# Expert stage of a fused attention and mixture-of-experts kernel: the loop over two rounds of four experts becomes eight bodies, with slot counts read ahead and with loads that wait for their own buffer

## What is computed

```python
def _moe2_ref(x, w_skip, w_gate, w1, w2):
    do_compute = x @ w_skip > 0
    out = x.copy()
    xc = x[do_compute]
    logits = xc @ w_gate
    e_idx = np.argmax(logits, axis=1)
    ...
    for e in range(E):                       # E = 8
        mask = e_idx == e
        h = np.maximum(xc[mask] @ w1[e], 0.0)      # w1[e]: 384 x 1024
        y[mask] = gate_w[mask, None] * (h @ w2[e]) # w2[e]: 1024 x 384
    out[do_compute] = xc + y
```

## Time and profile before

| | |
|---|---|
| median of 3 runs | 970.22 us (968.25 to 970.82) |
| the profiled execution's own time | 968.83 us |
| its span | 966.9 us |
| TensorE busy (matmuls) | 751.7 us, 78% of the span |
| VectorE busy | 699.2 us, 72% |
| ScalarE busy | 367.4 us, 38% |
| mean granted clock of TensorE | 0.922 of full speed |
| each w1 or w2 load of the expert stage | 1536 KB |
| first load of the expert stage issued | 766.68 us into the span |
| first and last start of an expert slot | 805.06 and 951.08 us |

### The profile page before, as it was taken

The page is one execution under the profiler, slowest core; times in us unless marked ns, Lnnn a source line. Parts: engine busy times, 40 slices in busy tenths (PEclk is TensorE's granted clock), DMA queues, the critical chain, the costliest instruction groups (busy, mean ns, idle before and its releaser), DMA issues. The chain is left out here.

```text
span 966.9 us, 16131 instructions
## 1 busy us (share of the span) xinstructions
PE 751.7 (78%) x5478; PEld 723.3 (75%) x5479; DVE 699.2 (72%) x1231; ACT 367.4 (38%) x805; POOL 51.8 (5%) x48
## 2 busy tenths in 40 slices
PE   1343456987897989889798889979999547998786
PEld 1333456987886989788688788879999447998786
DVE  6967988988999799898899989875333373434333
ACT  5452234435434534433453353334433222322221
POOL 1000000000000000000000000000000012233122
PEclk9999567999999899999999999999999857999799
DMA  6542343243342424424242352233210393324520
GB/s 188 178 152 79 93 118 90 64 130 113 80 109 62 139 65 115 126 66 133 70 118 73 100 151 63 70 113 97 57 56 1 133 357 110 126 73 163 205 82 17
DMA packets 82433, 104.74 MB, mean 108 GB/s; under 512 B 15990, under 2 KB 68384, under 8 KB 82336
## 3 DMA queue, kind: packets, MB, share of 16 engines
q1 hardware_dynamic: 80544, 99.69, 35.2%
q0 software_dynamic: 1792, 3.76, 1.2%
HBM read 61.04 MB, written 12.19 MB: 76 GB/s over the span
## 5 line engine op out<-in xcount | busy, mean ns | idle before, releaser
L524 PE MATMUL out_ps<-w_out_hi,g_parts 128*128 128x394 f32 x768 | 225.3, 350 | 26.3 <-DVE g_parts L933 26.3
L514 PE MATMUL mlp_ps<-xT,w_in_hi 128*128 128x384 f32 x768 | 207.1, 351 | 20.3 <-DMA xT<-y_parts 8.6
L524 PEld LDWEIGHTS out_ps<-w_out_hi,g_parts 128*128 128x128 f32 x768 | 145.9, 193 | 30.3 <-DVE g_parts L933 30.2
L514 PEld LDWEIGHTS mlp_ps<-xT,w_in_hi 128*128 128x128 f32 x768 | 140.5, 194 | 27.5 <-issue 13.5
L928 DVE SCALAR_TENSOR_TENSOR g<-mlp_ps,slope_side,bent 128x384 f32<-128x384 f32 x128 | 78.6, 615 | 83.4 <-ACT bent L666 75.3
L524 PE MATMUL out_ps<-w_out_lo,g_parts 128*128 128x394 f32 x384 | 133.8, 348 | 0.0
L514 PE MATMUL mlp_ps<-xT,w_in_lo 128*128 128x384 f32 x384 | 131.2, 342 | 0.0
L666 ACT ACTIVATE bent<-mlp_ps,bend_size 128x384 f32<-128x384 f32 x128 | 73.7, 576 | 149.5 <-PE mlp_ps L514 149.0
L1303 PE MATMUL mlp_ps<-xT_e,w_sb 128*128 128x128 f32 x624 | 79.5, 290 | 19.3 <-issue 14.1
L1303 PEld LDWEIGHTS mlp_ps<-xT_e,w_sb 128*128 128x128 f32 x624 | 77.4, 205 | 22.1 <-issue 16.9
L672 ACT ACTIVATE g_parts<-g 128x384 fp32r<-128x384 f32 x128 | 66.2, 517 | 35.4 <-DVE g L928 35.4
(11 more groups left out here) (150 smaller groups left out, 1082.8 us busy)
## 6 DMA issues: line engine op xcount, KB each, us to landing
kq<-qk_dec SPq DMA_DIRECT2D x96, 144.0 KB, 3.0
w_sb<-in_w SPq DMA_DIRECT2D x8, 1536.0 KB, 7.7
w_raw<-in_w SPq DMA_DIRECT2D x8, 1536.0 KB, 12.0
gates<-in_a SPq DMA_DIRECT2D x24, 384.0 KB, 4.3
qk_raw<-in_qk SPq DMA_DIRECT2D x24, 384.0 KB, 4.2
xT<-y_parts SPq DMA_DIRECT2D x48, 144.0 KB, 2.8
v_nat<-in_v SPq DMA_DIRECT2D x24, 192.0 KB, 4.0
out<-x SPq DMA_DIRECT2D x8, 576.0 KB, 3.2
```

Of the source, the lines that this page charges most:

```text
L514: last = pe.matmul(ps[:, 0:HT], w_in_v[s][:, kk, f * P:(f + 1) * P], xT[n.p][:, kk, m, :], start=(kk == 0 and j == 0), stop=(kk == KT - 1 ...
L524: last = pe.matmul(out_ps[i][:, 0:DL], g_parts[:, f % 4, s, i * P:(i + 1) * P], w_out_v[m][:, f, :], start=(f == 0 and j == 0), stop=(f == ...
```

## The change

The loop over i is gone: `for e in range(EXPERTS)` in Python writes out eight bodies on each engine. All eight slot counts are read into registers ahead of the first expert. TensorE no longer raises `expert_done`; VectorE raises `expert_left` at the end of each expert, when it has made that expert's last `y`. On SyncE the w2 load of a second-round expert is issued ahead of its w1 load and waits for `w2_lo` alone; the w1 load waits for `expert_left` of the expert whose buffer it overwrites.

```diff
-        def expert(x, i, p):
-            if isinstance(i, int):
-                return x[BODY * i + p:BODY * i + p + 1]
-            return x[bass.ds(i * BODY + p, 1)]
-        def slots_of(eng, i, p):
-            return eng.value_load(slots_i[0:1, bass.ds(i * BODY + p, 1)], min_val=0, max_val=NJ)
+        def expert(x, e):
+            return x[e:e + 1]
+        def slots_of_all(eng):
+            return [eng.value_load(slots_i[0:1, e:e + 1], min_val=0, max_val=NJ) for e in range(EXPERTS)]
...
-            def load(i, p):
-                if i > 0:
-                    sp.wait_ge(expert_done, i * BODY + p - (BODY - 3))
-                    sp.wait_ge(w1_loaded[p], 16 * i)
-                sp.dma_start(w1_v[p][:, :, :], expert(w1, i, p).rearrange("e (k p) f -> p (e k) f", p=P)).then_inc(w1_loaded[p], 16)
-                if i > 0:
-                    sp.wait_ge(w2_lo, i * BODY + p - (BODY - 1))
+            def load_w1(e):
+                p = e % BODY
+                if e >= BODY:
+                    sp.wait_ge(expert_left, e - BODY + 1)
+                    sp.wait_ge(w1_loaded[p], 16 * (e // BODY))
+                sp.dma_start(w1_v[p][:, :, :], expert(w1, e).rearrange("e (k p) f -> p (e k) f", p=P)).then_inc(w1_loaded[p], 16)
+            def load_w2(e):
+                p = e % BODY
+                if e >= BODY:
+                    sp.wait_ge(w2_lo, e - BODY + 1)
                 sp.dma_start(w2_raw[p][:, :, :],
-                             expert(w2, i, p).rearrange("e (f p) d -> p (e f) d", p=P)).then_inc(w2_loaded[p], 16)
-            for p in range(BODY - 1):
-                load(0, p)
+                             expert(w2, e).rearrange("e (f p) d -> p (e f) d", p=P)).then_inc(w2_loaded[p], 16)
+            for e in range(BODY - 1):
+                load_w1(e)
+                load_w2(e)
             sp.wait_ge(table_full, 1)
-            load(0, BODY - 1)
-            for i in range(1, EXPERTS // BODY):
-                for p in range(BODY):
-                    load(i, p)
+            load_w1(BODY - 1)
+            load_w2(BODY - 1)
+            for e in range(BODY, EXPERTS):
+                load_w2(e)
+                load_w1(e)
+            for p in range(BODY):
+                sp.wait_ge(w1_loaded[p], 16 * (EXPERTS // BODY))
...
-            until = pe.alloc_register("pe_slot_of_expert_before")
-            pe.reg_mov(until, 1)
             pe.wait_ge(slots_known, 1)
+            slots_here = slots_of_all(pe)
             pe.wait_ge(x_gathered, 16)
             turn_x()
...
-                pe.wait_ge(b_done, pe.snap(until, min_val=1, max_val=NSLOT - 1))
-                pe.sem_inc(expert_done, 1)
-                pe.reg_mov(until, count)
-            with pe.Fori(0, EXPERTS // BODY) as i:
-                for p in range(BODY):
-                    expert_slots(i, p)
+            for e in range(EXPERTS):
+                expert_slots(e)
...
-            def split(i, p):
-                if not (isinstance(i, int) and i == 0):
-                    act.wait_ge(expert_done, i * BODY + (p - 1))
-                act.wait_ge(w2_loaded[p], val(i * 16 + 16))
+            def split(e):
+                p = e % BODY
+                if e >= BODY:
+                    act.wait_ge(expert_left, e - BODY + 1)
+                act.wait_ge(w2_loaded[p], e // BODY * 16 + 16)
                 act.activation(w2_v[p][0][:, :, :], w2_raw[p][:, :, :], ACT.Copy).then_inc(w2_hi, 1)
             count = act.alloc_register("act_slot")
             act.reg_mov(count, 1)
-            split(0, 0)
-            split(0, 1)
+            split(0)
+            split(1)
+            act.wait_ge(slots_known, 1)
+            slots_here = slots_of_all(act)
             place_x(1)
-            act.wait_ge(slots_known, 1)
-            def expert_slots(i, p):
-                n = slots_of(act, i, p)
+            def expert_slots(e):
+                n = slots_here[e]
                 def split_next():
-                    if p < BODY - 2:
-                        split(i, p + 2)
-                    else:
-                        with act.If(i < EXPERTS // BODY - 1):
-                            split(i + 1, p + 2 - BODY)
-                        act.nop()
+                    if e + 2 < EXPERTS:
+                        split(e + 2)
...
+                dve.sem_inc(expert_left, 1)
```

More of the change, by code:

```diff
@@ L1195, in phase2 @@
         w2_lo = sem("w2_lo")
-        expert_done = sem("expert_done")
+        expert_left = sem("expert_left")
         x_gathered = sem("x_gathered")
@@ L1284, in _ @@
             pe.reg_mov(count, 1)
-            until = pe.alloc_register("pe_slot_of_expert_before")
-            pe.reg_mov(until, 1)
             pe.wait_ge(slots_known, 1)
+            slots_here = slots_of_all(pe)
             pe.wait_ge(x_gathered, 16)
             turn_x()
-            def expert_slots(i, p):
-                n = slots_of(pe, i, p)
+            def expert_slots(e):
+                n, p, i = slots_here[e], e % BODY, e // BODY
                 def slot(is_first=False):
@@ L1297, in slot @@
                     if is_first:
-                        pe.wait_ge(w1_loaded[p], val(i * 16 + 16))
+                        pe.wait_ge(w1_loaded[p], i * 16 + 16)
                     for g in range(NP):
@@ L1310, in slot @@
                     if is_first:
-                        pe.wait_ge(w2_hi, val(i * BODY + (p + 1)))
-                        pe.wait_ge(w2_lo, val(i * BODY + (p + 1)))
+                        pe.wait_ge(w2_hi, e + 1)
+                        pe.wait_ge(w2_lo, e + 1)
                     for f in range(NFE):
@@ L1385, in expert_slots @@
                 act.nop()
-                with act.If(n < 1):
-                    split_next()
+                if e + 2 < EXPERTS:
+                    with act.If(n < 1):
+                        split_next()
+                        act.nop()
                     act.nop()
-                act.nop()
                 over_slots(act, n, slot)
-            with act.Fori(0, EXPERTS // BODY) as i:
-                for p in range(BODY):
-                    expert_slots(i, p)
+            for e in range(EXPERTS):
+                expert_slots(e)
         @block.vector
@@ L1510, in keep_x, with split @@
                 dve.tensor_copy(x_kept_rows[:, bass.ds(s % 2, 1), :].rearrange("p a d -> p (a d)"), x_in[:, :]).then_inc(x_kept, 1)
-            def split(i, p):
-                dve.wait_ge(w2_hi, val(i * BODY + (p + 1)))
+            def split(e):
+                p = e % BODY
+                dve.wait_ge(w2_hi, e + 1)
                 dve.tensor_tensor(w2_v[p][1][:, :, :], w2_raw[p][:, :, :], w2_v[p][0][:, :, :].bitcast(F32), ALU.subtract).then_inc(w2_lo, 1)
@@ L1521, in _ @@
             dve.tensor_copy(scatter_at[:, :], tab[:, NSLOT - 1, 0:1]).then_inc(first_at, 1)
-            split(0, 0)
+            split(0)
+            dve.wait_ge(slots_known, 1)
+            slots_here = slots_of_all(dve)
             keep_x(1)
@@ L1525, in _, with expert_slots @@
             dve.reg_mov(count, 1)
-            dve.wait_ge(slots_known, 1)
             dve.wait_ge(step, val(last_step))
-            def expert_slots(i, p):
-                n = slots_of(dve, i, p)
+            def expert_slots(e):
+                n = slots_here[e]
                 def split_next():
[L1533 to L1538, removed]
+                    if e + 1 < EXPERTS:
+                        split(e + 1)
                 def slot(is_first=False):
@@ L1563, in expert_slots @@
                 dve.nop()
-                with dve.If(n < 1):
-                    split_next()
+                if e + 1 < EXPERTS:
+                    with dve.If(n < 1):
+                        split_next()
+                        dve.nop()
                     dve.nop()
-                dve.nop()
                 over_slots(dve, n, slot)
-            with dve.Fori(0, EXPERTS // BODY) as i:
-                for p in range(BODY):
-                    expert_slots(i, p)
+                dve.sem_inc(expert_left, 1)
+            for e in range(EXPERTS):
+                expert_slots(e)
         @block.gpsimd
         def _(pool):
-            pool.sem_inc(expert_done, 1)
             pool.sem_inc(b_done, 1)
```

## The result

The changed kernel takes 956.74 us (median of 4 runs, 954.14 to 957.86) against 969.41 for the kernel before in the same comparison: a ratio of 0.9877 with a 95% interval from 0.9848 to 0.9906. It is faster by 12.7 us (9.1 to 14.7 by that interval), where 19.7 were forecast (970.22 to 950.5); the time lies 0.7 us above the forecast range.

A forecast was written before the change was run, and what follows sets the result against it. TensorE bounds the 13 slots (busy 137.67 of 156.40 us); 1.98 + 1.0 + 6.10 + 2.73 + 5.15 + 3 x 1.02 − 0.7 = 19.3 us off 968.83 gives 949.5, the median 1.4 higher: 950.9, stated as 950.5, range 946.5 to 956.

The forecast's parts named there:

- Loads of w2: Second-round w2 loads come 15 us or more early; gaps inside slots 5, 8, 11 go: 1.98, about 1.0, slot 11 separately.
- The loop's branch: Behind slot 8, TensorE's 6.58 us passage shrinks to 0.48: 6.10 us, plus 2.73 for slot 9's first layer at full clock.
- The end of each expert: Wait, increment and count go from TensorE's passages: 1.02 us each where the sequencer is late, counted for slots 3, 9, 12.
- The far jumps stay: TensorE's jumps over unused bodies at experts' ends remain, each passage kept as it was, 3.46 us over three bodies.
- Slot 11: Without the wait and slow matmuls it takes 11.08 instead of 16.23 us: 5.15 gained, including its own 1.02.
- The counts ahead: Eight slot-count reads before the first expert, 5.4 us on each engine, are hidden by other waits: nothing taken.
- The first, a fetch that stays: Rival: the loop branch's 4.90 us moves to expert 4's entry, losing 4.9 + 2.7 us, time 958; chance 0.08.
- the second: Rival: expert 4's w2 delays the first gather, awaited by slot 1, some 4 us once or twice: 954 to 958; chance 0.08.
- the clock was low only behind idle times: Rival: TensorE's clock is lowered for being busy without gaps, 5.5 us more per slot, 972 to some 1004; chance 0.03.
- no split waits any more: Rival: ScalarE's splits waited for expert_done, not the load, so gaps stay: some 5 us less gain, 955.5; chance 0.04.
- signs of being wrong: Idle over 2 us ahead of slot 9 or 10, first gather landing after 804, or transposes awaiting gathers in several slots.
- The rule of the Trainium skill: Code comes in 256-instruction blocks; jumps outside a two-block window wait: expert 5's turns short, 0 short, 3 long, 1 us more.

The follow-up runs named there:

- loop_new_loads: The kernel before, with its loop and counts in place, given the new loads only (w2 first, w1 told by VectorE): 965.42 us, ratio 0.9999.
- counts_in_place: Changed kernel with each slot count read at the start of its expert on the three engines, as before: 958.90 us, one run.
- pad40: Changed kernel with 40 increments of an unused semaphore on TensorE ahead of expert 0, moving expert code by 39 places: 954.25 us, ratio 0.9874.
- pad140: Changed kernel with 140 semaphore increments on TensorE ahead of expert 0: 967.0 us, one run.
- calm: Changed kernel, SyncE alone altered: expert 5's w2 issued ahead of expert 4's w1, which waits until expert 1 is left: 955.20 us, ratio 0.9886.
- old_loads: Changed kernel's eight bodies and counts ahead, but second-round loads in the order and with the waits of before: 960.57 us, ratio 0.9938.
- paced_pad40: pad40 with second-round loads one by one, each held until the next slot's gather has landed: 949.47 us, ratio 0.9817.
- late_pair: calm with expert 6's w1 and expert 7's w2 held until seven slots are done: 957.18 us, one run.
- paced2: Changed kernel with loads held one by one for gathers, in another order than paced_pad40's, no increments added: 953.13 us, ratio 0.9840.
- paced2_pad40: paced2's loads with the 40 increments on TensorE: 948.19 us, ratio 0.9803.

## Why the prediction was wrong

By its own steps, against the changed kernel's slots:

- **Loads of w2: right in mechanism and in place.** All were issued within some 3 us of the forecast, the gaps in slots 5, 8 and 11 are gone. In loop_new_loads, though, the loads alone gain nothing that the time shows (ratio 0.9999), because of what follows.
- **The loop's branch: right.** Slots 8 and 9 take 10.68 and 10.90 us where 10.8 and 10.83 were worked out; 10.9 us gained.
- **The end of each expert: right but for the jumps.** 1.02 us a passage, of which 0.67 is the count's; counts_in_place puts back 0.66 to 0.89 for that part once its jumps' own differences are taken off.
- **"The far jumps stay": this is the step that failed.** They stayed in number, but their price was taken from an execution in which no load was in flight at them, and the same change moved loads onto one. Slots 3 and 4 were worked out at 11.08 and 10.7 us (with the 0.7 for the gather, a wait that no run here shows in slot 4) and took 13.82 and 12.55: 4.6 us lost. In the five kernels with loads in flight there (changed, pad40, pad140, loop_new_loads, counts_in_place) the jump took 6.16 to 6.42 us; in the five with none (before, calm, old_loads, paced_pad40, late_pair) 3.42 to 3.74; in the two paced2 kernels, where the end of one w1 load reaches into it (12.2% and 9.3% of the DMA engines' time), 3.88 and 4.66. The prediction asked what the earlier loads collide with, and looked at gathers alone.
- **Slot 10 was not in the sum.** 10.02 us expected as before, 13.65 measured: 3.6 us, 1.75 of them a stop of the sequencer, the rest slow matmuls. The prediction used the place of the code for the jumps over two bodies alone and did not ask how far behind a jump's target the next block begins. pad40, pad140 and paced2 show that the stop belongs to the place, and the packets that it is the wait for the next block.
- **Slot 11 was 1.2 us better:** 9.92 against 11.08, since expert 5's jump was short.
- **The counts ahead: right.** They cost nothing on any engine.

4.6 + 3.6 − 1.2 = 7.0 us, and the slots took 144.0 us where the sum gave 136.9; slots 1 and 12, 0.3 shorter and 0.4 longer, are the rest. None of the rivals was the cause. The first, a fetch that stays, was near in kind but put at expert 4's entry, where the gap is 0.60 us; the second had the weights collide with the first gather, but its transposes ran at 803.4 as before (and its price, 4 us for a load alone, was low: in paced_pad40 w1 loads issued alone landed 6.3 to 6.7 us after their issue); the clock was low only behind idle times; and no split waits any more. Of what the prediction called signs of being wrong none came, but the clock was not at 1.00 from slot 2 on: it was 0.50 behind slot 3.

The rule of the Trainium skill ("Runtime: NRT & Kernel Launch", "Instruction fetch mechanics") did better on the jumps than the sum, which kept them as they were: by the count of places expert 0 and 5 short and 3 long, which the trace shows with 344, 752 and 3338 ns, and in pad140 all three the other way. It does not hold throughout: in calm, with the same code, expert 5's jump took 3555 ns with no weights in flight, and paced2_pad40's case is above. What decides there stays open. The section also says that crossing a block is mostly hidden; slot 10's stop of 1.75 us is a case where it isn't. That weights delay a fetch agrees in kind with what the Trainium skill's "DMA: Bandwidth & Descriptors" ("Queues, rings and completion order") says, that each DMA engine takes turns between the queues that have work: the fetch starts 3.55 to 3.75 us after the jump instead of 0.9 to 1.3. Why the wait is that long is not shown.

## What to carry to other kernels

Before loads are moved earlier, list everything else that uses the DMA engines in the new place, and TensorE's own instructions are one such thing: a jump whose price was read in a quiet stretch isn't priced for a busy one. A stall that one engine causes can also be what kept a load away from another wait; here the loop's branch kept the loads of expert 6 off the next far jump, as old_loads shows. The change gave 12.7 us, the same code with loads spaced out 14.8, and with 40 increments as well 19.7; only the last is clear of the first by its interval. Where code is written out, look at the stretch right behind each long jump: 40 cheap instructions in a time of waiting were worth 4.4 us in the slots of the changed kernel and 2.2 with the loads spaced out, by one traced execution each, and such tuning holds for one routing and one layout of the code.

## What the runs showed of the hardware

- A far jump of TensorE's sequencer took 3.3 to 3.9 us in a quiet stretch, up to 4.75 us where two instruction packets overlapped, and 6.16 to 6.42 us with two 1536 KB loads in flight. It ended 1.3 to 1.7 us after its instruction packet of 16 KB (64 of 65 jumps); what the loads changed is when that packet starts, 3.55 to 3.75 us after the jump instead of some 1.0.
- Behind a far jump TensorE could stop once more, for 0.84 to 2.57 us within a slot, until 1.43 to 1.57 us after the next instruction packet.
- An idle of 3.74 us was followed by a granted clock of 0.50 and a first layer of 8.15 us. For shorter idles it varied: after 1.75 us inside slot 10 the remaining 40 matmuls took 6.33 us in the changed kernel and 4.73 in calm, with the same idle of 1.75.
- Semaphore increments on TensorE took some 0.15 us each: with 140 of them the first slot began 12 us late, while 40 fitted into the wait for the first gather.
